# A second MoE that routes 24 tiles of tokens by token number: rows and logits of the first MoE scattered, and x's low parts made on VectorE

## The reference, cut to what matters

```python
def _moe_ref(x, modality_id, w_gate, modality_bias, w1, w2):
    logits = x @ w_gate + modality_bias[modality_id]
    e_idx = np.argmax(logits, axis=1)
    ...
        out[mask] = gate_w[mask, None] * (np.maximum(x[mask] @ w1[e], 0.0) @ w2[e])

def _moe2_ref(x, w_gate, w1, w2):
    cap = N // E                                  # 3072 // 8 = 384
    logits = x @ w_gate
    order = np.argsort(-logits.flatten())
    for idx in order:
        tok, e = (int(idx) // E, int(idx) % E)
        if assigned[tok] >= 0 or counts[e] >= cap:
            continue
        assigned[tok] = e
        counts[e] += 1
    ...
        out[mask] = np.maximum(x[mask] @ w1[e], 0.0) @ w2[e]      # D = 512, F = 1024
```

## Time and profile before

| | us |
|---|---|
| median of three runs | 1154.97 |
| the three runs | 1154.97, 1146.36, 1155.27 |
| the profiled execution | 1148.96 |
| its span in the trace | 1146.9 |

### The profile page before, as it was taken

One profiled execution on the slowest core, in us unless ns is written; L12 is line 12 of the kernel. 1 busy time (PEld: TensorE's weight loads), 2 busy tenths in 40 slices (PEclk: granted clock), 3 DMA queues, 4 the chain that ended last, 5 costly groups with the idle time before them and its releaser, 6 DMA issues.

```text
span 1146.9 us, 22896 instructions
## 1 busy us (share of the span) xinstructions
PE 1011.8 (88%) x7214; PEld 867.6 (76%) x7215; DVE 489.9 (43%) x1488; ACT 460.8 (40%) x1034; POOL 491.7 (43%) x462
## 2 busy tenths in 40 slices
PE   5999999997599999989999983369999999988796
PEld 4899888986488888878888863357878787787685
DVE  3766767676511122231122237854755546440000
ACT  4767676765322222242222230123434343343441
POOL 7454444441120000140000140437776687877882
PEclk9999999998599999999999995569999999998998
DMA  8556565651531111151111110423243332335300
GB/s 208 146 136 158 139 154 132 152 137 35 205 144 37 37 37 37 37 183 37 37 37 37 37 37 1 172 77 102 102 159 118 130 103 101 111 106 183 107 28 28
DMA packets 57403, 113.57 MB, mean 99 GB/s; under 512 B 6672, under 2 KB 23056, under 8 KB 57360
## 3 DMA queue, kind: packets, MB, share of 16 engines
q1 hardware_dynamic: 51280, 92.98, 26.6%
q0 software_dynamic: 6080, 19.98, 5.5%
HBM read 91.37 MB, written 21.57 MB: 98 GB/s over the span
## 4 chain that ended last, share of the span: by engine, by line
PE 49%; POOL 14%; issue 13%; DMA 8%; DVE 7%; ACT 4%; DVEq 4%; POOLq 1%; SPq 0%; ACTq 0%
DMA out<-sb_rows_out,sb_tokens_at 6%; PE ps_bank L855 5%; PE ps_bank L837 4%; PE ps_bank L839 4%; PE ps_bank L838 4%; PE ps_bank L856 4%; POOL sb_w2l L566 4%; PE ps_bank L857 4%; POOL sb_hl L634 4%; PE ps_bank L727 3%; PE ps_bank L716 3%; PE ps_bank L744 2%; PE ps_bank L746 2%; PE ps_bank L762 2%; DVEq L1241 2%
## 5 line engine op out<-in xcount | busy, mean ns | idle before, releaser
L1442 DVE TENSOR_TENSOR sb_hl<-ps_bank,sb_hh 128x512 fp32r<-128x512 f32 x52 | 35.7, 687 | 227.8 <-ACT sb_hh L1111 227.8
L555 POOL COPY sb_gather_at<-sb_slot_token_i 128x1 int32 (+1 forms) x27 | 4.9, 182 | 278.6 <-PE ps_bank L816 278.6
L1041 ACT ACTIVATE sb_probs<-sb_masked,sb_neg_max 128x260 f32<-128x260 f32 (+1 forms) x192 | 94.4, 492 | 67.0 <-DVE sb_neg_max L1228 63.9
L566 POOL TENSOR_TENSOR sb_w2l<-sb_w_raw,sb_w2h 128x1024 fp32r<-128x1024 f32 x44 | 107.5, 2453 | 16.3 <-ACT sb_w2h L1097 16.3
L518 POOL TENSOR_TENSOR sb_kl<-sb_k_raw,sb_kh 128x768 fp32r<-128x768 f32 x32 | 58.6, 1833 | 122.2 <-ACT sb_kh L1054 122.1
L984 PE MATMUL ps_bank<-sb_xh,sb_w1h 128*128 128x384 f32 x256 | 97.0, 379 | 9.9 <-ACT sb_h L1167 7.9
L623 POOL TENSOR_TENSOR sb_w1l<-sb_w_raw,sb_w1h 128x1024 fp32r<-128x1024 f32 x32 | 75.6, 2378 | 39.3 <-ACT sb_w1h L1092 39.2
L1228 DVE CUSTOM_DVE_ANT_0 sb_masked<-ps_bank,sb_mask 128x260 f32<-128x260 f32 (+1 forms) x192 | 75.8, 401 | 34.4 <-PE ps_bank L716 31.4
L837 PE MATMUL ps_bank<-sb_w1h,sb_xh 128*128 128x512 f32 x208 | 83.4, 401 | 7.9 <-DVE sb_w1l L1431 6.2
L855 PE MATMUL ps_bank<-sb_w2h,sb_hh 128*128 128x512 f32 x208 | 86.3, 415 | 3.7
L985 PE MATMUL ps_bank<-sb_xl,sb_w1h 128*128 128x384 f32 x256 | 89.0, 348 | 0.0
(11 more groups left out here) (298 smaller groups left out, 2706.6 us busy)
## 6 DMA issues: line engine op xcount, KB each, us to landing
sb_w_raw<-w1b SPq DMA_DIRECT2D x8, 2048.0 KB, 8.7
sb_w_raw<-w2b SPq DMA_DIRECT2D x8, 2048.0 KB
sb_q_raw<-qT SPq DMA_DIRECT2D x64, 192.0 KB, 3.6
sb_k_raw<-kT SPq DMA_DIRECT2D x64, 192.0 KB, 3.8
y_rows<-sb_y_out SPq DMA_DIRECT2D x34, 258.0 KB, 2.4
sb_v<-v_tiles SPq DMA_DIRECT2D x32, 192.0 KB
x_rows<-sb_x_pair SPq DMA_DIRECT2D x16, 384.0 KB, 3.7
sb_w_raw<-w1a SPq DMA_DIRECT2D x3, 2048.0 KB, 8.8
```

The lines of the kernel that those rows point to most:

```text
L566: pool.tensor_tensor(w2_part(w2l, p), w2_part(raw2, p), w2_part(w2h, p).bitcast(F32), ALU.subtract).then_inc(w2_lo[m], 1)
L1041: act.activation(probs[g % 2][:, 0:width(g)], masked_scores[g % 2][:, 0:width(g)], ACT.Exp, bias=neg_max[g % 2][:], scale=-1.0, accum_out= ...
```

## The change

The second MoE works by token number. The tables of the second routing have `NT` = 24 tiles. Token t stands in partition t // 24, column t % 24, and what comes out of a phase are token numbers, with which both the gather and the scatter of the second MoE work.

1. First MoE: SP stores no tile any more. POOL scatters each tile's rows to `y_dram` by token, and each tile's logits (8 floats for a token) to a new `l_dram`; empty slots go to spare rows behind them. Behind the last tile SP waits for the last logits' landing and loads all logits back into SBUF in one DMA, for which DVE waits. The stores of zeros to `y_dram` at the start of the program go.
2. Second routing: 24 tiles in all DVE operations and PE's counts, `choice2` is kept with the expert innermost, and `step_places` and the places of the transposes are new (the triples in the calls of `expert_products`: a transpose of the next expert's tile stands behind that place of the down product, counted from 0).
3. Second MoE: `low_x` moves from POOL to DVE (in `give_out`) and reads PSUM, so ACT's plain copy of x goes. `low_h` moves to DVE for the last two experts (`FREE = E - 2` is the first of them), with ACT's plain copy of h. `keep_tokens`, `landed` and the copy of the slots leave POOL. `copy_y` on ACT waits for the scatter of two tiles before. `gather` of the next expert stands ahead of the last two `low_h`. ACT's and POOL's loops over experts are written out.

```diff
+    y_dram = nc.dram_tensor("y_rows", (N + SPARE, DM), F32, kind="Internal").ap()
+    l_dram = nc.dram_tensor("y_logits", (N + SPARE, E), F32, kind="Internal").ap()
...
 @block.sync
-                    sp.wait_ge(y_copied, t + 2)
-                    sp.wait_ge(token_put, t + 2)
-                    sp.dma_start(y_dram[bass.ds(t * P, P)], y_rows[:]).then_inc(y_stored, 16)
+            sp.wait_ge(l_stored, tiles * 16 + 32)
+            settle(sp)
+            sp.dma_start(logits2[:], l_dram[0:N].rearrange("(p t) e -> p t e", t=NT)).then_inc(logits2_loaded, 16)
...
 @block.gpsimd
+            def note_places(t):
+                pool.wait_ge(y_stored, t * 16 + 16)
+                pool.wait_ge(l_stored, t * 16 + 16)
+                settle(pool)
+                pool.tensor_copy(put_at[:], out_i[:, bass.ds(t, 2)])
+                pool.tensor_copy(gather_at[:], slot_token_i[:, bass.ds(t + 2, 1)]).then_inc(at_copied, 1)
+                pool.wait_ge(at_copied, t + 2)
...
                 with pool.Fori(first, end) as t:
-                    gather_x(t + 2)
+                    note_places(t)
+                    fetch_x(t + 2)
+                    scatter_logits(t)
+                    scatter_y(t)
...
+            pool.wait_ge(logits2_kept, tiles + 2)
+            settle(pool)
+            put_logits(put_at[:, 1:2])
...
                 for f in range(FC):
-                    low_h(k, f)
+                    if f == FC - 2 and not last:
+                        gather(k + 1)
+                    if k < FREE:
+                        low_h(k, f)
                     if f < WP:
                         low_w2(1, k, f)
                 if not last:
-                    gather(k + 1, 1 - a)
                     low_w1(k + 1, 0)
                     low_w1(k + 1, 1)
-                    keep_tokens(k + 1, 1 - a)
                     low_w1(k + 1, 2)
-                scatter(k, a, 0)
+                scatter(k, 0)
                 if not last:
-                    low_x(k + 1, 0)
                     low_w1(k + 1, 3)
-                    low_x(k + 1, 1)
-                landed(k, 0)
-                scatter(k, a, 1)
-                if not last:
-                    low_x(k + 1, 2)
-                landed(k, 1)
-                scatter(k, a, 2)
-                landed(k, 2)
+                scatter(k, 1)
+                scatter(k, 2)
...
 @block.tensor
-                for t in range(half * MT // 2, (half + 1) * MT // 2):
-                    mm = pe.matmul(r_ps[0:TRIES[s], 0:E], passed[:, t, 0:TRIES[s]], choice2[:, :, t],
+                for t in range(half * NT // 2, (half + 1) * NT // 2):
+                    mm = pe.matmul(r_ps[0:TRIES[s], 0:E], passed[:, t, 0:TRIES[s]], choice2[:, t],
...
-            step_places = [0, 1, 5, 8, 10, 14, 17, 19, 24, 25, 27, 29, 31, 33, 34, 36, 38, 39, 41, 46, 51]
+            step_places = [3, 4, 7, 9, 10, 14, 16, 17, 22, 23, 24, 25, 28, 30, 31, 33, 35, 36, 38, 43, 50]
...
-            expert_products(E - 4, 0, True, False)
-            expert_products(E - 3, 1, False, False)
-            expert_products(E - 2, 0, False, False)
+            expert_products(E - 4, 0, True, (8, 9, 14))
+            expert_products(E - 3, 1, False, (5, 6, 8))
+            expert_products(E - 2, 0, False, (3, 5, 7))
...
 @block.scalar
             def high_x(k, i):
                 act.wait_ge(xp2_ready, k * CT + i + 2)
-                act.wait_ge(x2_lo, k * CT + i + 1)
-                act.copy(xh[:, :, i * P:(i + 1) * P], h2_ps[i % 2][:].rearrange("p (c n) -> p c n", c=DC))
-                act.copy(x32[:], h2_ps[i % 2][:]).then_inc(x2_hi, 1)
+                act.copy(xh[:, :, i * P:(i + 1) * P], h2_ps[i % 2][:].rearrange("p (c n) -> p c n", c=DC)
+                         ).then_inc(x2_hi, 1)
...
-                act.wait_ge(scattered, k * CT + i + 1)
+                if k * CT + i >= 2:
+                    act.wait_ge(out_stored[at], (k * CT + i) // 2 * 16)
...
 @block.vector
+            dve.wait_ge(logits2_loaded, 16)
+            L2 = logits2[:]
...
+            def low_x(k, i):
+                dve.wait_ge(x2_hi, k * CT + i + 1)
+                cols = slice(i * P, (i + 1) * P)
+                dve.tensor_tensor(xl[:, :, cols], h2_ps[i % 2][:].rearrange("p (c n) -> p c n", c=DC),
+                                  xh[:, :, cols].bitcast(F32), ALU.subtract).then_inc(x2_lo, 1)
...
+                if not first:
+                    low_x(k - 1, 0)
+                    low_x(k - 1, 1)
                 dve.wait_ge(ties_ranked, k + 1)
...
                 run_mine()
+                if not first:
+                    low_x(k - 1, 2)
```

332 lines of the change are left out of this document (181 added, 151 removed).

## The result

The changed kernel takes **1099.59 us** (median of four runs, 1098.62 to 1100.51) where the kernel before takes 1151.35 beside it (four runs, 1146.36 to 1155.27): a ratio of 0.9553, with a 95% interval of 0.9504 to 0.9601. The profiled executions, 1148.96 and 1098.62 us, are 50.3 us apart.

What follows compares the result with a forecast made beforehand. DVE's chain bounds the second routing's phases 0 and 1, PE experts 0 to 4; in experts 5 and 6 PE waits for gathered rows. Terms summed to -28.9 from 1148.96, giving 1120 us, range 1104 to 1138.

Steps and rivals of the forecast that it cites:

- The hop: Logits through DRAM between first MoE and second routing: scatter, load and wakes, covered by nothing, add 6.8 us.
- Phases 0 and 1: Second routing's first phases: shorter DVE operations and PE counts, choice2 without a stride, save 10.3 us.
- Experts 5 to 7: Last experts of the second MoE: terms -4.5, -3.7 and -2.0 us, with gathers held up by the 2 MB load.
- The counts: Second MoE's routing counts on PE: 0.4 us for a count, 1.6 us saved an expert in experts 1 to 4.
- The slower rival: First MoE: POOL's loop takes 18.4 us a tile for PE's 15.0, making the whole 1208 us; chance 0.06.
- First MoE, taken as 0: First MoE: PE and ACT hide POOL's new scatters, so its time changes by 0, bounds -1 and +5 us.
- the zero stores that go lie beside the loads of attention: Program start: removing the stores of zeros gains nothing, counted within the 0 for the first MoE.
- The 1.63 us of 'issue' at PE's loop ..., stay, as PE's loop does: PE's gap from expert 1 to 2 stays, within the -11 us for experts 1 to 4.
- I gave 1.5 back for the low clock: Expert 0: products fill formerly idle time at low clock, so 1.5 us comes back, leaving 49.7 us, -4.2.
- POOL's 46.6 us of waits give PE nothing here.: Experts 1 to 4: POOL's 46.6 us of waits for scatters to land end in time, so PE gains nothing.

Runs made afterwards that it cites:

- e11: Changed kernel with POOL's wait for x's gathered rows moved behind the tile's two scatters: 1097.16 us.
- e13: Changed kernel with four more matmuls in each half of a count, so that a half has 16 as before: 1110.50 us.
- e7: Kernel before with choice2 stored by tile, so that DVE writes it without a stride, 32 tiles kept: 1146.08 us, ratio 0.9881.
- e14: Changed kernel where SP starts the 2 MB load of w2b for experts 6 and 7 only when that expert's gathered rows have landed: 1088.21 us.
- e1: Changed kernel with SP's eight early stores of zeros and POOL's last wait for scatters, with a small memset, put back: 1101.12 us.
- e2: Kernel before, with POOL's w2 subtractions waiting for DVE's four of w1 at expert changes in the first MoE: 1148.53 us, ratio 0.9948.
- e15: The kernel of e13 (counts of 16) with PE's loop over two pairs of experts written out: 1106.95 us.
- e3: Changed kernel with the list of step places of the kernel before: 1102.38 us.
- e8: Changed kernel where POOL again waits for each of its scatters to land before it goes on: 1107.63 us.
- e6: Kernel before with POOL's and ACT's loops over the pairs of experts written out, nothing else: 1151.52 us, ratio 0.9978.
- e5: Kernel before with the changed kernel's list of step places: 1145.85 us, ratio 0.9907.

## Why the prediction was wrong in size and right in sign

**What held.** *The hop*: +6.6 for +6.8, by luck, as the parts are others: the transfers took 4.1 us where I had 6.2; the wakes and issues, my 0.2, 0.3 and 0.1 for which no row stood, took 1.0; and 1.5 us were a wait I hadn't seen, of DVE for the row of logits before. e11 takes it away. The Trainium skill (DMA: Bandwidth & Descriptors, section on the anatomy of one DMA on the SWDGE path) gives a DMA from POOL about 2.0 us plus its bytes at 436 GB/s, and the trace agrees: the scatter took 2.1 us. I had used that price for the load too, which SP issues; it took 2.0. *Phases 0 and 1*: -9.8 for -10.3, again better in the sum than in its parts: PE's shorter counts, 2.4 us in my sum, are worth 1.0 by e13, and `choice2`, 1.6 in my sum, 1.1 by e7 (last copy of y to expert 0, 70.3 for 71.3). *Experts 5 to 7*: -9.7 for -10.2; the gathers land late because of the load, as I had it (the last landings 27.8 and 23.6 us into the experts for my 28 and 24), which e14 shows by moving the load alone. *The counts*: 0.40 us for one on PE, as I said. *The slower rival*: the tiles of the first MoE keep 13.97 us, so POOL's loop doesn't bound them.

**The step that failed first: "First MoE, taken as 0".** It is two things. I wrote that "the zero stores that go lie beside the loads of attention"; they lay ahead of them on SP's queue, and e1 prices them at 1.7 us of the 2.2 that were won by the first copy of y. At the changes of expert I costed only what POOL and DVE gained or lost in work. The change delays POOL's first w2l by the issue of one scatter, and that took DVE's subtraction out of its way: 6.0 us, by e2, of which 1.6 are half clock behind one of the two waits and not there in every execution. The row was in the trace before: the longest of twelve like instructions was 2.8 times the median, and PE waited 6.2 us for the group.

**The step that failed second: "The 1.63 us of 'issue' at PE's loop ..., stay, as PE's loop does".** The loop stays but its body gets shorter, and by e13 and e15 that is what the gap hangs on. With it went the half clock behind it. In the kernel before, experts 1 to 4 hold two stretches at half clock, which cost 2.9 us together by the starts of the products in them, the gap of 1.6, and 3.7 us of waits for thresholds; I had taken away only the last. These and 7.2 us of counts make 15.4 of the 17.4; some 2 us are spread over the steps and I don't settle them. Of the 1.6 us for the counts of an expert the fewer matmuls are 1.3 by e13. The rest is the order of `choice2`: with 16 tiles a half, an expert's counts take 6.23 us by the starts of PE's instructions before and 5.89 in e7 (expert 3 in both). In expert 0 the wait of 3.8 us for thresholds went, as I had it, but I gave 1.5 back for the low clock, and the clock came out at 0.96 for 0.90 instead. That e3 also gives 3.9 us for the places is chance: there the wait is 2.3 us and the rest is half clock.

**The step that was not in the sum: the end.** I wrote nothing of what lies behind PE's last matmul. POOL's last wait stood ahead of the program's end there; without it the end comes 1.9 us sooner (e1, e8). Another 2.1 us by the spans come with the change, as POOL's DRAIN is shorter by so much. Their cause stays open: POOL's and ACT's loops are not the reason (e6).

**"POOL's 46.6 us of waits give PE nothing here."** Right for experts 0 to 4 as the change is (e8), and not the whole of it: with the new places and POOL as before, PE waits for x's low part at each expert (e5). That suggests that the last 3 us there (0.5 to 1.0 an expert) need both the places and x's low part on DVE; the second alone was not tried.

**The range** ended at 1104 (by its own terms, 1111 less 2, 3 and 1, at 1105). It took its low end from rivals and bounds inside the steps that I had, and had no room for a stage that I had set to 0 with bounds of -1 and +5. The stage gave -8.2.

## What to carry to other kernels

In a group of like instructions compare the longest with the median before you call a stage unchanged: behind an operation at 2.8 times its median look for a partner on another engine, as a change that shifts this partner by a microsecond can move the path. Issue gathers whose rows PE waits for ahead of the next large load, not beside it, and let the load wait for them: that alone was 10 to 11 us here, a fifth of what the whole change brought. A long loop body on PE can be fetched again at each turn, and here that cost up to 2.7 us and the clock behind it; look at "issue" at the loop's edge, and shorten the body or write it out.

## What the runs showed of the hardware

- DVE's subtraction of two SBUF tiles takes 1.22 us alone and 3.40 when POOL's like subtraction has started first, and POOL's takes 3.37 for 2.38 behind DVE's; DVE's subtraction of h, which reads PSUM, keeps its 0.69 us beside POOL's (499.19 in the changed kernel, POOL in w2l from 494.02).
- POOL's issue of the scatter takes 1.73 us at both changes of expert, beside DVE's subtraction of two SBUF tiles, and 0.97 to 1.01 in other tiles. The cause isn't shown: beside the same subtractions a gather's issue took 1.00 us in the changed kernel (306.1) and 0.98 in the kernel before (308.7).
- At PE's jump back over two experts' code, with 411 to 419 matmuls an expert, it stood for 1.6 to 2.7 us in four profiles and for 0.35 to 0.99 in three, and the code was fetched again; with 363 it never stood, and nothing was fetched.
- In the profiles with a wait of 1.0 to 2.2 us that ended at 24 to 25 us (e2, e6, e7), PE's granted clock was 0.50 for the next 14 to 17 us; a wait of 0.55 us there left it at 1.00. Later waits of 1.14 us (811.90 and 910.60 in the kernel before) left it at 1.00 too.
- A gather of three times 256 KB lands 2.7 and 3.8 us later beside a 2 MB load: the waits of PE behind it are 5.75 and 4.07 us with the load and 3.08 and 0.31 without.
